# Which operand stands still: the token-mixing down projection of a fused attention and mixer kernel, with x stationary and U's 32 columns moving

## What is computed

```python
def _moe_ref(x, U, V, w_ch1, w_ch2):          # x: 2 x 768 x 512, U: 768 x 32, V: 32 x 768
    xt = x.transpose(0, 2, 1)
    h = xt @ U @ V                              # mixes the 768 tokens through rank 32
    u = x + h.transpose(0, 2, 1)
    ch = np.maximum(u @ w_ch1, 0.0) @ w_ch2     # 512 -> 2048 -> 512
    return (u + ch).astype(np.float32)
```

## Time and profile before

| | |
|---|---|
| median of 3 runs | 652.67 us (652.26 to 653.36) |
| the profiled execution's own time | 654.16 us |
| its span, first to last instruction | 652.4 us |
| mean granted TensorE clock | 0.997 |
| TensorE busy | 635.1 us (97%) |
| its weight loads busy | 569.2 us (87%) |
| VectorE, ScalarE, GpSimd busy | 331.6, 318.3, 366.7 us |

### The profile page before, as it was taken

The page is one execution under the profiler, slowest core; times in us unless marked ns, Lnnn a source line. Parts: engine busy times, 40 slices in busy tenths (PEclk is TensorE's granted clock), DMA queues, the critical chain, the costliest instruction groups (busy, mean ns, idle before and its releaser), DMA issues.

```text
span 652.4 us, 10391 instructions
## 1 busy us (share of the span) xinstructions
PE 635.1 (97%) x3554; PEld 569.2 (87%) x3554; DVE 331.6 (51%) x718; ACT 318.3 (49%) x723; POOL 366.7 (56%) x373
## 2 busy tenths in 40 slices
PE   8999999999999999999999999999999999999997
PEld 7888798899889897899999988889999888899986
DVE  6776542333343344377667662186668325676411
ACT  5657565445444453564445444464444455444321
POOL 8545456556555565356756654475756543757262
PEclk9999899999999999999999999999999999999999
DMA  7344254343333415123232333233233343421142
GB/s 174 94 95 118 46 146 131 98 129 81 92 80 89 159 52 162 50 80 99 80 113 81 102 104 101 82 113 97 81 114 96 91 139 94 146 86 45 49 136 90
DMA packets 88420, 65.51 MB, mean 100 GB/s; under 512 B 43024, under 2 KB 72464, under 8 KB 88368
## 3 DMA queue, kind: packets, MB, share of 16 engines
q1 hardware_dynamic: 88368, 64.85, 35.1%
HBM read 61.42 MB, written 3.15 MB: 99 GB/s over the span
## 4 chain that ended last, share of the span: by engine, by line
PE 87%; DVE 4%; POOL 3%; issue 3%; ACT 2%; DVEq 0%; ACTq 0%; POOLq 0%
PE bank L1383 33%; PE bank L1177 21%; PE bank L1349 10%; PE bank L1239 4%; PE bank L1212 4%; PE bank L1220 3%; PE bank L1313 3%; PE bank L1276 3%; PE bank L1257 2%; PE bank L1290 1%; PE bank L1197 1%; POOL w_lo L764 1%; ACT w_hi L785 1%; PE bank L1375 1%; DVE masked L971 1%
## 5 line engine op out<-in xcount | busy, mean ns | idle before, releaser
L764 POOL TENSOR_TENSOR w_lo<-w_raw,w_hi 128x512 fp32r<-128x512 f32 (+1 forms) x158 | 205.7, 1307 | 172.2 <-ACT w_hi L785 171.8
L785 ACT ACTIVATE w_hi<-w_raw 128x512 fp32r<-128x512 f32 (+1 forms) x158 | 96.4, 618 | 61.8 <-PE bank L1383 42.7
L1177 PE MATMUL bank<-b_hi,a_hi 128*128 128x384 f32 x280 | 94.8, 338 | 1.0 <-DVE temps L1083 0.7
L1177 PE MATMUL bank<-b_lo,a_hi 128*128 128x384 f32 x280 | 94.8, 339 | 0.0
L1383 PE MATMUL bank<-w_hi,hid_hi 128*128 128x512 f32 x216 | 87.6, 406 | 0.0
L1383 PE MATMUL bank<-w_hi,hid_lo 128*128 128x512 f32 x216 | 85.1, 394 | 0.0
L1383 PE MATMUL bank<-w_lo,hid_hi 128*128 128x512 f32 x216 | 84.7, 392 | 0.0
L817 ACT ACTIVATE probs<-masked,neg_max 128x264 f32<-128x264 f32 x96 | 49.5, 515 | 67.3 <-DVE neg_max L971 66.9
L1383 PE MATMUL bank<-w_hi,y_hid 128*128 128x512 f32 x216 | 71.0, 394 | 0.2
L971 DVE CUSTOM_DVE_ANT_0 masked<-bank,masks 128x264 f32<-128x264 f32 x96 | 41.1, 430 | 38.5 <-PE bank L1212 34.0
L915 DVE SCALAR_TENSOR_TENSOR hid_lo<-bank,hid_hi 128x384 fp32r<-128x384 f32 x32 | 17.8, 557 | 78.2 <-ACT hid_hi L773 78.2
(11 more groups left out here) (142 smaller groups left out, 1415.0 us busy)
## 6 DMA issues: line engine op xcount, KB each, us to landing
w_raw<-in_moe_w_ch_dram SPq DMA_DIRECT2D x144, 256.0 KB, 2.8
w_raw<-in_moe_w_ch_dram SPq DMA_DIRECT2D x20, 512.0 KB, 3.5
q_nat<-in_q_dram SPq DMA_DIRECT2D x12, 256.0 KB, 3.0
k_nat<-in_k_dram SPq DMA_DIRECT2D x12, 256.0 KB, 3.7
v_nat<-in_v_dram SPq DMA_DIRECT2D x12, 256.0 KB, 3.3
out_dram<-o_stage SPq DMA_DIRECT2D x11, 256.0 KB, 3.5
w_raw<-in_moe_w_tok_dram SPq DMA_DIRECT2D x6, 256.0 KB, 2.6
w_raw<-in_moe_w_tok_dram SPq DMA_DIRECT2D x8, 192.0 KB, 2.3
```

The lines of the kernel that those rows point to most:

```text
L764: nc.gpsimd.tensor_tensor(w_lo[:, split % NW, 0:n], w_raw[:, split % NR, 0:n], w_hi[:, split % NW, 0:n].bitcast(f32), ALU.subtract) \
L785: nc.scalar.activation(w_hi[:, split % NW, 0:n], w_raw[:, split % NR, 0:n], ACT.Copy) \
L1177: last = mm(bank[:, 0:HALF], w[at % 2][:, a, k, :], u[:, b_part, k, :], start=(first and n == 0), stop=(n == 5), skip_group_check=True)
```

## The change

The operands of "down" change places. U is loaded once (`U_sb`, 32 columns) and moves; the stationary operand is a block of 128 tokens by 128 columns of x, four blocks per tile (KD = 4). The sum over the tiles is low^T, 128 x (4 x 32) in one bank. After the last tile ScalarE writes the rounded values twice into `low_T` (blocks of 3 x 32 columns: high, low, high), VectorE the low part between them. A new step "downT" transposes the four blocks of 128 x 96 back on TensorE, and VectorE copies the 96 x 512 result into `low3`. From there on all is as before. In the plan "downT" stands right behind the last "down" of batch 0, and for batch 1 it is a unit of its own in `preparation(1, 1)`; `waiting` has 67 units with it and is used up at the 64th place.

```diff
--- before.py
+++ after.py
@@ -143,7 +143,7 @@
     def preparation(layer, b):
 
         if layer == 1:
-            units = [[("down", 1, b, 2 * c), ("down", 1, b, 2 * c + 1)] for c in range(NQ // 2)]
+            units = [[("down", 1, b, 2 * c), ("down", 1, b, 2 * c + 1)] for c in range(NQ // 2)] + [[("downT", 1, b)]]
         else:
             split = [[("xsplit", b, 2 * c), ("xsplit", b, 2 * c + 1)] for c in range(NQ // 2)] + [[]]
             units = [split[0]] + [[("down", 2, b, c)] + split[c + 1] for c in range(NQ // 2)]
@@ -180,7 +180,7 @@
 
 
     BUSY_BEFORE = {("qT", 0): 8, ("qT", 1): 10, ("scores", 0): 4}
-    plan = [s for unit in attention(0) for s in unit] + [("down", 1, 0, NQ - 1)]
+    plan = [s for unit in attention(0) for s in unit] + [("down", 1, 0, NQ - 1), ("downT", 1, 0)]
     waiting = attention(1) + preparation(1, 1)
     for n, s in ((24, ("wload", 0)), (23, ("wload", 1)), (19, ("wsum", 0)), (16, ("wsplit", 0)), (11, ("wsum", 1)),
                  (11, ("wload", 2))):
@@ -191,7 +191,7 @@
         if s[0] in ("mm1", "mm2", "up") and waiting and not (s[0] == "mm2" and ends(s)):
             n += 1
             plan += waiting.pop(0)
-            if n % 16 == 0:
+            if n % 16 == 0 and waiting:
                 plan += waiting.pop(0)
     assert not waiting
     plan += seven(1, 1, preparation(2, 0)) + seven(2, 0, preparation(2, 1)) + seven(2, 1, [])
@@ -254,7 +254,10 @@
             his_at[key] = len(his_at)
 
     for s in plan:
-        if s[0] == "down":
+        if s[0] == "downT":
+            open_bank((("down",) + s[1:], 1), DOWN_BANKS[s[1:]][0])
+            close_bank((("down",) + s[1:], 1), False)
+        elif s[0] == "down":
             for g in range(1 if s[1] == 1 else KG):
                 if s[3] == 0:
                     open_bank((s[:3], g), DOWN_BANKS[s[1:3]][g])
@@ -293,7 +296,8 @@
 
         ident = sb("ident", [P, P])
         x_nat = sb("x_nat", [P, B, NQ, DM])
-        U3_sb = sb("U3_sb", [P, NQ, 3 * RANK])
+        U_sb = sb("U_sb", [P, NQ, RANK])
+        low_T = sb("low_T", [P, KD, 3, RANK], f32r)
         V3_sb = sb("V3_sb", [3 * RANK, S], f32r)
         low3 = sb("low3", [3 * RANK, DM], f32r)
         with ExitStack() as before_u:
@@ -629,9 +633,7 @@
                 sp.dma_start(sink_raw[N_SINK * h:N_SINK * (h + 1), :, D * h:D * (h + 1)],
                              v[:, h, 0:N_SINK, :].rearrange("b j d -> j b d")).then_inc(vsink_loaded, 16)
             load_v(1)
-            for n in range(3):
-                sp.dma_start(U3_sb[:, :, n * RANK:(n + 1) * RANK],
-                             moe_U.rearrange("(t p) r -> p t r", p=P)).then_inc(U_loaded, 16)
+            sp.dma_start(U_sb[:, :, :], moe_U.rearrange("(t p) r -> p t r", p=P)).then_inc(U_loaded, 16)
             sp.wait_ge(vsink_loaded, 16 * H)
             for n in range(1, 3):
                 sp.dma_start(sink_raw[HS * n:HS * (n + 1)], sink_raw[0:HS]).then_inc(vsink_copied, 16)
@@ -834,7 +836,11 @@
                     act.wait_ge(probs_ready, H * (T + 1))
                     nc.scalar.add(sums_eps[:, T % 2, :], sums[:, T % 2, :], 1.0e-9).then_inc(eps_added, 1)
                 elif s[0] == "down" and s[1] == 1 and s[3] == NQ - 1:
-                    high_of((s[:3], 0), 3 * RANK, low3[:, :], ACT.Copy)
+                    key = (s[:3], 0)
+                    act.wait_ge(m_ready, m_at[key] + 1)
+                    src = m_tile(key)[:, 0:KD * RANK].rearrange("p (d r) -> p d r", d=KD)
+                    nc.scalar.activation(low_T[:, :, 0:3:2, :], src.unsqueeze(2).broadcast_to([P, KD, 2, RANK]),
+                                         ACT.Copy).then_inc(hi_ready, 1)
                 elif s[0] == "down" and s[1] == 2 and s[3] == NQ // 2 - 1:
                     for g in range(KG):
                         high_of((s[:3], g), P, tok_hi[:, g, :], ACT.Relu)
@@ -1005,8 +1011,15 @@
                         nc.vector.tensor_tensor(part, V3_raw[2 * RANK:3 * RANK, :], part.bitcast(f32),
                                                 ALU.subtract).then_inc(V_split, 1)
                 elif s[0] == "down" and s[1] == 1 and s[3] == NQ - 1:
-                    rows = slice(RANK, 2 * RANK)
-                    low_of((s[:3], 0), rows, low3[rows, :], low3[rows, :])
+                    key = (s[:3], 0)
+                    dve.wait_ge(hi_ready, his_at[key] + 1)
+                    src = m_tile(key)[:, 0:KD * RANK].rearrange("p (d r) -> p d r", d=KD)
+                    nc.vector.tensor_tensor(low_T[:, :, 1, :], src, low_T[:, :, 0, :].bitcast(f32),
+                                            ALU.subtract).then_inc(m_drained, 1)
+                elif s[0] == "downT":
+                    key = (("down",) + s[1:], 1)
+                    dve.wait_ge(m_ready, m_at[key] + 1)
+                    nc.vector.tensor_copy(low3[:, :], m_tile(key)[0:3 * RANK, :]).then_inc(m_drained, 1)
                 elif s[0] == "down" and s[1] == 2 and s[3] == NQ // 2 - 1:
                     for g in range(KG):
                         low_of((s[:3], g), every, tok_lo[:, g, :], tok_hi[:, g, :], relu=True)
@@ -1251,13 +1264,24 @@
                     _, layer, b, t = s
                     use = (s[:3], 0)
                     if t == 0:
-                        pe.wait_ge(U_loaded, 48)
+                        pe.wait_ge(U_loaded, 16)
                         m_free(use)
                     pe.wait_ge(x_ready, NTILES if b else t + 1)
-                    last = mm(m_tile(use)[0:3 * RANK, :], U3_sb[:, t, :], x_nat[:, b, t, :],
-                              start=(t == 0), stop=(t == NQ - 1), skip_group_check=True)
+                    for d in range(KD):
+                        last = mm(m_tile(use)[:, d * RANK:(d + 1) * RANK], x_nat[:, b, t, d * P:(d + 1) * P],
+                                  U_sb[:, t, :], start=(t == 0 and d == 0), stop=(t == NQ - 1),
+                                  skip_group_check=True)
                     if t == NQ - 1:
                         last.then_inc(m_ready, 1)
+                elif s[0] == "downT":
+                    wait_out((("down",) + s[1:], 0))
+                    use = (("down",) + s[1:], 1)
+                    m_free(use)
+                    for d in range(KD):
+                        last = nc.tensor.transpose(m_tile(use)[0:3 * RANK, d * P:(d + 1) * P],
+                                                   low_T[:, d, :, :].rearrange("p c r -> p (c r)").bitcast(f32),
+                                                   ident[:, :])
+                    last.then_inc(m_ready, 1)
                 elif s[0] == "down":
                     _, layer, b, c = s
                     pe.wait_ge(wlo_ready, chunk_at[s] + 1)
@@ -1295,7 +1319,7 @@
                     for d in range(KD) if first else s[4:]:
                         transposes(d)
                     if first or s[4] == 0:
-                        wait_out((("down", layer, b), 0 if layer == 1 else KG - 1))
+                        wait_out((("down", layer, b), KG - 1))
                     if layer == 1:
                         pe.wait_ge(V_split, 1)
                     elif s[4] == 0:
```

## The result

The changed kernel takes 655.70 us, the median of six runs (655.33 to 656.98), beside 652.46 us for the kernel before on the same chip (652.12 to 653.36). The ratio is 1.0049, with a 95% interval of 1.0037 to 1.0062: slower by 3.2 us, where the prediction said 4.5. Its profiled execution took 656.98 us, with a span of 655.2 and a mean granted clock of 0.995.

The account below looks back on a forecast made before the run. TensorE was taken as the bound, busy 635.1 of 652.4 us. Passes +0.4, batch 0 +2.6, downT +0.4 and plan +1.1 made +4.5 on 652.67, so 657.2 us, range 654.3 to 659.6.

Parts of the forecast that it names:

- passes: Twelve down steps: eight short passes of 0.111 us replace two wide ones per step, +0.4 us, between -2.2 and +0.7.
- turn of batch 0, full clock: Between batch 0's last down step and up: TensorE idles for low_T, then sixteen transposes, +1.1 us if the clock returns.
- the clock: Batch 0's turn: the lower clock level lasts through the sixteen transposes, 1.5 us of that turn's +2.6.
- "downT" of batch 1: Four more transposes on TensorE, +0.4 us, with the wait for low_T hidden behind a mixer slot.
- plan, the stall: Second s2 product of (1, 1) waits for VectorE's sum as up comes a slot later, +1.1 us, bounds 0 and 1.4.
- plan, wsum one slot later: First pairs' wsum, wsplit and wload come a slot later; their reader s1 is several slots on, cost nothing.
- Rival D: Down passes: loads hide, a short pass costs 0.055 us, twelve steps save 5.0, time 651.8; chance 0.05.
- Rival A: Batch 0's turn: the clock comes back as in the kernel before, 655.7 us; chance 0.18.
- rival C: More of the lower clock, 1.7 us over the forecast, 658.9 us; chance 0.12.
- Rival B: No stall in s2, VectorE's idle bits giving back 1.4 us; 656.1 us; chance 0.13.
- A and B together: Clock back as before and no s2 stall, 654.6 us; chance 0.09, shared with load and stream in turn.

Follow-up runs that it names:

- e9: e3 plus sixteen unread identity transposes, eight in TensorE's wait for batch 0's last x and eight ahead of batch 0's downT; 652.66 us, ratio 1.0019.
- e1: The kernel before with only wsum 1 and wload 2 attached one unit later in the list; 650.91 us, ratio 0.9979.
- e3: The changed kernel with batch 1's down steps three to a unit, keeping the plan's length, and wsum behind the last x; 654.17 us, ratio 1.0026.
- e2: The kernel before with an empty unit where the change puts downT, and no new down step; 652.58 us, ratio 1.0002.
- after: The changed kernel itself, all edits in, against the kernel before; 655.70 us, ratio 1.0049.
- e4: The changed kernel with U's 32 columns streamed four times per pass, 128 moving columns instead of 32; 656.73 us, ratio 1.0059.
- e6: e3 with only batch 0's down steps turned and batch 1's as in the kernel before; 654.39 us, ratio 1.0028.
- e7: e3 with nine of the twelve x transposes of batch 0's first up step issued ahead of downT; 653.99 us, ratio 1.0022.
- e8: e1 plus eight unread identity transposes while TensorE waits for the last x of batch 0; 651.0 us, ratio 0.9978.
- e10: e7 plus e8's eight identity transposes ahead of batch 0's last down step; 653.44 us, ratio 1.001.
- e5: e3 with only batch 1's down steps turned and batch 0's as in the kernel before; 651.78 us, ratio 0.9992.

## Why the prediction was right, and where it was wrong

The sign, the range and the mechanism hold: short passes that cost as much as the wide ones they replace, an uncovered "downT", a stall in s2 from the longer plan. The size is 1.3 us off, and that has one main place, the last line but one of the table.

| term | predicted | measured, and where |
|---|---|---|
| passes | +0.4 | +0.4 (0.2 in five attention steps, 0.2 in batch 1) |
| turn of batch 0, full clock | +1.1 | +0.93 at the first mm1, 1.16 at "up" (e9 against e1) |
| the clock | +1.5 | +1.5 (e3 against e9) |
| "downT" of batch 1 | +0.4 | +0.4 (0.59 in the table, less 0.2 of passes) |
| plan, the stall | +1.1, bounds 0 and 1.4 | +1.5 in medians, 1.7 to 1.8 in traces (e2, e3, after) |
| plan, wsum one slot later | 0 | -1.3 (e1) |
| sum | +4.5 | +3.4 with 0.93 and 1.5 of these, beside 3.2 in the medians |

**The step that failed** is "wsum, wsplit and wload of the first pairs come a slot later too; their reader is s1 at 287.54, several slots on, so they cost nothing". That they cost nothing is right. But the step asked only who reads them, not what stood behind them on their own engine: x of the last tile, for which TensorE was seen to wait 1.2 us (e1 shows the cause). A delayed instruction also frees its place in the queue.

**The passes.** 0.112 us where 0.111 was predicted, and e4 shows that the moving columns do not set it: the row of the nearest shape was the right guide. Rival D, the loads that hide, is refuted by the same spacing. By the Trainium skill ("TensorE: Matmul & The Clock Gate", LDWEIGHTS), a load takes its columns over 1.2 GHz, an estimate of 107 ns for these 128. The spacing of the passes agrees with it within 5 ns; the load's own duration in the profile does not, it is 191 ns.

**The turn.** The wait was 0.89 us for 0.9. In after's profiled execution "downT" began 1.97 us after the last down step (77.58 - 75.61), not 2.8 (78.0 - 75.21), because that step's passes ran at the full level, in 1.08 us and not the 2.02 of the earlier trace rows. In e6's, where they ran at the lower level, it was 2.81 (77.19 - 74.38).

**The clock: right in size by luck.** The prediction had the low stretch begin where it began before and last through sixteen transposes, to 81.4, 6.2 us after the start of the last down step. In after's profiled execution it did not. It began at 78.1, behind the gap; the four of "downT" still ran at the full level (0.11 each), and those of x at half. So in the profiled pair the turn lost 1.09 us up to "up" and 1.34 up to mm1, not 2.6; the second low stretch, at 47.4, took the rest. But the predicted picture does occur: in the profiled executions of e4, e6 and e7 the turn's low stretch lasted 6.8 us, and the turn took 6.23, 6.08 and 5.51 us, in e4 and e6 close to the 6.2. What was wrong in every case is the base, which was taken for a kernel with a low stretch. Its profiled execution has one; the median one has none: of 76 executions 57 have a mean clock of 0.999 or more. After the change no execution is without one: none of 39 of the five kernels with narrow passes in batch 0 and no transposes of ident laid in (after, e3, e4, e6, e7). So the 1.5 us is not the step from a low stretch to a longer one but that from none to one that always comes, and at times comes twice or lasts twice as long; that the two differences are of one size is chance.

Rival A (the clock comes back as now: 655.7) has the right time by chance too, since what brought 657.2 down was wsum. Behind rival C stood a rule of the Trainium skill ("TensorE: Matmul & The Clock Gate", Part 4, PE-mode transpose): the full clock does not engage for transposes. The trace of after does not agree: in the start-up it engaged with nothing but transposes on TensorE. e8 and e9 point the same way: waits filled with transposes alone, and the executions with a fall went from 3 of 11 to none and from 10 of 10 to 5 of 11, though small numbers and another chip stand in the way of calling that shown. The prediction read the same from the kernel before, where it does not quite follow: there the clock rose at 10.0, 0.2 us after the first matmul that is no transpose.

**The stall.** Mis-sized, above its upper bound. The work of the last "up" unit on VectorE came 2.05 us later against s1 (282.93 - 279.82 = 3.11, less 1.06), for the 2.1 predicted, and with 0.7 in hand that gives 1.4. But VectorE did not catch up, it fell back further: three low parts of T (L1067) took 3.78 us, where the same three took 3.27 before. A subtraction of GpSimd (1.86 us from 287.30) now lies wholly beside them; before, it met them only in part and took 1.56. The traces of e2 and e4, which have the stall, show the same two durations within 0.01, and those of e1, e3 and e9, which don't, show 3.27 and about 1.56; a single low part takes 0.96 us, and a subtraction that meets none of them 1.28. That the two engines slow each other where they overlap fits all of these; no run isolates it. Rival B, no stall, is refuted by after and e2.

**Small slips in the working.** The range's lower end is said to be A and B together, which is 654.6 and not 654.3; the upper end of the passes' term, +0.7, has no working; and (0.49 - 0.27) / 2 is 0.110, not 0.108. None of them moves the forecast.

**Left open.** Why the clock also fell at 47 to 51 us, just behind the third narrow down step, in three of the seven profiled kernels with narrow passes in batch 0 (after, e7, e10) and in none of the five profiled with wide ones (before, e1, e2, e5, e8). In these three the clock had first risen at 6.4 to 7.8 us, in the other four narrow ones at 5.0 to 5.8; but it had risen at 7.1 in e1 and 6.5 in e8 too, without a fall. So the narrow passes are the suspect, and when the clock first rose seems to decide too; no run took the narrow passes alone out of the attention and left all else. Nor did a narrow kernel without the added transposes run on the chip of e9 and e10.

## What to carry to other kernels

Turning a product round so that the narrow operand moves gains nothing once a pass no longer gets shorter with its columns (here from 128 down): count passes, not streamed columns, and take the price from the nearest product with the same stationary shape. A step that is added to a hand-made order moves everything behind it, so ask of each moved instruction both who reads it and what stood behind it in its engine's queue; an empty step in the old kernel measures the order's share by itself. And when a stage has short waits on a busy TensorE, look at the clock in many executions, not in the profiled one alone.

## What the runs showed of the hardware

- A plain fp32 pass with 128 stationary columns costs 0.112 us with 32 moving columns and with 128 (after, e4), and 0.111 with 64.
- On one core the clock's fall is a matter of chance in each execution: the same kernel had it in 19 of 76 executions and not in the others, some 1 us apart (mostly up to 652.7 without, from 652.9 with it), and in 2 of 21 on one chip, 17 of 55 on two others. With short passes about the waits of 0.9 us it came in 39 of 39, and the medians moved by 1.5 us.
- Transposes alone can lift the clock: in after it rose at 6.4 us, the first other matmul came at 8.55.
- Eight transposes of 0.11 us that nobody reads, laid into a wait of 0.9 us, cost nothing that can be seen (the last down step starts 52.51 us after the first tile's product in e8, 52.52 in e1), and the falls became rarer (0 of 11 in e8, 11 of 22 in e9 and e10), with the doubts named above.
- Where a subtraction of GpSimd (128x512, 1.28 us away from them) lay wholly beside three of VectorE's (128x768, 0.96 for a single one), they took 1.86 and 3.78 us (after, e2, e4); where it overlapped them in part, 1.56 and 3.27.
